# Four groups ahead and four buffers in the attention ahead of two feed-forward stages, with the guard of the row sums on GpSimd

## The reference

```python
k_sum = k.reshape(B, H, nb, block, D).max(axis=3)
v_sum = v.reshape(B, H, nb, block, D).mean(axis=3)
scores_l = where(|i - j| < 16, scale * q @ k.T, -1e9)
scores_s = scale * q @ k_sum.T + log(32)
a = exp(all - max(all)); a = a / (sum(a) + 1e-9)
x = a @ concat(v, v_sum)                 # 1536 tokens x 512
x = relu(x @ w_in) ** 2 @ w_out          # 512 -> 2048 -> 512
h = x @ w2_in
out = (P(h) / (Q(h) + 1e-6)) @ w2_out    # P cubic in h; Q = 1 + |b0||h| + |b1|h*h
```

## Time and profile before

| | before |
|---|---|
| median of 3 runs | 616.96 us (616.08 to 617.96) |
| profiled execution, its own time | 617.14 us |
| its span | 615.4 us |
| PE busy | 582.0 us (95%), 3360 matmuls |
| DVE busy | 444.0 us (72%) |
| ACT busy | 261.3 us (42%) |
| GpSimd busy | 145.1 us (24%) |
| bytes moved | 32.68 MB, of them 0.34 and 0.08 of instructions |

### The profile page before, as it was taken

The page is one execution under the profiler, slowest core; times in us unless marked ns, Lnnn a source line. Parts: engine busy times, 40 slices in busy tenths (PEclk is TensorE's granted clock), DMA queues, the critical chain, the costliest instruction groups (busy, mean ns, idle before and its releaser), DMA issues.

```text
span 615.4 us, 9725 instructions
## 1 busy us (share of the span) xinstructions
PE 582.0 (95%) x3360; PEld 472.8 (77%) x3360; DVE 444.0 (72%) x834; ACT 261.3 (42%) x553; POOL 145.1 (24%) x150
## 2 busy tenths in 40 slices
PE   4788699999999999999999989999999999999995
PEld 3556578888888888888888867788888888888884
DVE  4678787665343233456675699999999999999996
ACT  3778611111031111311111855556766566766564
POOL 5556610000030000210000656522221222221220
PEclk9999999999999999999999999999999999999999
DMA  8788433000000000022333200000100000100001
GB/s 232 212 261 251 129 128 148 0 1 0 1 0 0 0 0 0 0 81 91 103 102 103 69 1 0 1 0 1 68 0 0 0 0 0 68 1 0 1 2 68
DMA packets 12351, 32.68 MB, mean 53 GB/s; under 512 B 1568, under 2 KB 3872, under 8 KB 12320
## 3 DMA queue, kind: packets, MB, share of 16 engines
q1 hardware_dynamic: 12320, 32.25, 16.8%
HBM read 27.92 MB, written 3.15 MB: 50 GB/s over the span
## 4 chain that ended last, share of the span: by engine, by line
PE 47%; DVE 36%; issue 9%; ACT 3%; DMA 2%; DVEq 1%; POOL 1%; SPq 1%; POOLq 0%
PE bank L499 22%; PE bank L544 21%; DVE ratio L927 9%; DVE numer L909 6%; DVE ratio L921 5%; DVE numer L907 5%; DVE ratio L916 5%; DVE hhi L934 4%; ACT prob L617 2%; DMA vwin<-vsum 2%; PE bank L468 1%; PE bank L449 1%; PE bank L485 1%; PE bank L459 1%; SPq L250 1%
## 5 line engine op out<-in xcount | busy, mean ns | idle before, releaser
L499 PE MATMUL bank<-xhi,whi 128*128 (+1 forms) x384 | 150.3, 391 | 0.3 <-DVE wlo L820 0.3
L499 PE MATMUL bank<-xlo,whi 128*128 (+1 forms) x384 | 149.9, 390 | 0.0
L499 PE MATMUL bank<-xhi,wlo 128*128 (+1 forms) x384 | 149.8, 390 | 0.0
L630 ACT ACTIVATE hsq<-bank 128x512 f32<-128x512 f32 x48 | 28.8, 600 | 218.5 <-PE bank L499 218.5
L409 POOL TENSOR_TENSOR denom<-denom,habs 128x512 f32<-128x512 f32 (+1 forms) x49 | 62.3, 1272 | 250.9 <-ACT denom L686 250.9
L499 PEld LDWEIGHTS bank<-xhi,whi 128*128 128x128 f32 x384 | 72.5, 189 | 15.9 <-DVE wlo L820 0.7
L499 PEld LDWEIGHTS bank<-xhi,wlo 128*128 128x128 f32 x384 | 72.3, 188 | 15.1
L499 PEld LDWEIGHTS bank<-xlo,whi 128*128 128x128 f32 x384 | 72.4, 189 | 14.9
L559 PE MATMUL bank<-whi,hhi 128*128 128x512 f32 x192 | 75.9, 395 | 7.6 <-DVE hlo L938 7.6
L559 PE MATMUL bank<-whi,hlo 128*128 128x512 f32 x192 | 74.8, 390 | 0.0
L559 PE MATMUL bank<-wlo,hhi 128*128 128x512 f32 x192 | 74.8, 389 | 0.0
(11 more groups left out here) (65 smaller groups left out, 858.9 us busy)
## 6 DMA issues: line engine op xcount, KB each, us to landing
wraw<-w SPq DMA_DIRECT2D x32, 512.0 KB, 4.1
vwin<-vw SPq DMA_DIRECT2D x8, 576.0 KB, 5.4
kraw<-kT SPq DMA_DIRECT2D x8, 400.0 KB, 6.0
q<-qT SPq DMA_DIRECT2D x8, 384.0 KB, 6.4
out<-osb SPq DMA_DIRECT2D x12, 256.0 KB, 2.1
vwin<-vsum SPq DMA_DIRECT2D x32, 36.0 KB
ca<-coef_a SPq DMA_DIRECT2D x1, 2.0 KB, 10.7
braw<-coef_b SPq DMA_DIRECT2D x1, 1.0 KB, 11.8
```

What stands on the lines that cost most here:

```text
L499: last = mm(hps[j % 2][:, :], W[a][:, j, kt * P:(kt + 1) * P], X[b][:, kt, bass.ds(CH * c, CH)], start=k == 0, stop=k == 3 * KT - 1)
```

## The change

The probability buffers are four, and PE's scores, DVE's masks and ACT's exponentials run four, four and three groups ahead rather than three, three and two. The guard goes from DVE to GpSimd and stands one group further ahead (`guard(G + 3)`), as do `invert(G + 2)`, still on DVE, and `normalise(G + 2)`. There are four buffers of value windows, and the order of SP's transfers is another one. Summaries are computed in the groups that `SUMMARY_AT` lists (1, 3, 5, 8, 11, 14, 17). Key rows are loaded without their zero edges, which DVE writes once, and key 0 comes in three parts. The means are built on ACT. The coefficients are loaded later. The first three weights are split by GpSimd in quarters (w_in part, from group 17 on) and by DVE (w_out part, in the last three groups), and the first two hidden tiles are computed in lots of six matmuls in each of the last four groups. Left out below: the parts of names and waits that only follow from the new counts.

```diff
-DVE_FIRST = 2
...
-P_RING = 3
+P_RING = 4
...
+V_RING = 4
...
+THIRD = S // GPB
+SPLIT_FROM = GROUPS - 7
+SUMMARY_AT = [0, 1, 3] + [GPB * n - 4 for n in range(3, NB)]
...
+    prob = [places[1](f"prob{i}", [P, GU, COLS]) for i in range(P_RING)]
...
-    prob = [area(f"prob{i}", [P, GU, COLS]) for i in range(P_RING)]
...
+    vwin.append(area("vwin3", [COLS, NW, P]))
...
-            sp.dma_start(kraw[n % RING][:, :], kT[n]).then_inc(k_in[n % RING], 16)
+            sp.dma_start(kraw[n % RING][:, BAND:BAND + S], kT[n]).then_inc(k_in[n % RING], 16)
+        def load_k_first(i):
+            sp.dma_start(kraw[0][:, BAND + THIRD * i:BAND + THIRD * (i + 1)],
+                         kT[0][:, THIRD * i:THIRD * (i + 1)]).then_inc(k_first[i], 16)
...
-        load_k(0)
+        load_k_first(0)
+        load_k_first(2)
         load_q(0)
+        load_vwin(0)
         load_k(1)
-        load_vwin(0)
         load_q(1)
+        load_k(2)
         load_vwin(1)
-        load_k(2)
         load_q(2)
-        sp.dma_start(ca[:, :], coef_a.partition_broadcast(P)).then_inc(coef_in, 16)
-        sp.dma_start(braw[:, :], coef_b.partition_broadcast(P)).then_inc(coef_in, 16)
-        spread_summary(0)
         for n in range(NB):
-            if n + 2 < NB:
-                load_vwin(n + 2)
+            if n == 0:
+                load_vwin(2)
+            elif n + RING < NB:
+                load_vwin(n + RING)
             if n + RING < NB:
                 load_k(n + RING)
+            if n == 0:
+                spread_summary(0)
+                load_vwin(RING)
+                spread_summary(1)
+            if n + RING < NB:
                 load_q(n + RING)
             if 2 <= n < 2 + EARLY:
                 load_first(n - 2)
+            if n == 5:
+                sp.dma_start(ca[:, :], coef_a.partition_broadcast(P)).then_inc(coef_in, 16)
+                sp.dma_start(braw[:, :], coef_b.partition_broadcast(P)).then_inc(coef_in, 16)
             if n >= 5:
                 for j in range(EARLY + 2 * (n - 5), min(EARLY + 2 * (n - 4), FT // 2)):
                     load_weights(w1, j, *landing(j))
-            if n + 1 < NB:
-                spread_summary(n + 1)
+            if n == 1:
+                spread_summary(2)
+            if 0 < n and n + 2 < NB:
+                spread_summary(n + 2)
...
+        def guard(G):
+            r = G % P_RING
+            pool.wait_ge(exp_done, G + 1)
+            g.tensor_scalar(guarded[r][:, :], rowsum[r][:, :], 1e-9, None, ALU.add).then_inc(guard_done, 1)
...
+        guard(0)
...
+        guard(1)
...
+        normalise(1, 1)
+        guard(2)
+        def split_in(x):
+            j, part = x // 2, SLOT // 4 * (x % 2)
+            index = slice(None), j, slice(part, part + SLOT // 4)
+            split(index, w_hi_pool, x, w_in_ready)
         for G in range(GROUPS):
...
-            if G + 1 < GROUPS:
-                normalise(G + 1, (G + 1) % P_RING)
-            if n + 2 < NB:
+            if G + 2 < GROUPS:
+                normalise(G + 2, (G + 2) % P_RING)
+            if G == 1:
+                load_windows(2)
+                spread_all(2)
+            if 1 <= n < NB - 2:
                 if gi == 0:
...
                 elif gi == 1:
...
-            x = G - GROUPS + 4
-            if x >= 0:
-                if x == 0:
-                    pool.wait_ge(w_first, 16 * EARLY)
-                if x < 2 * (EARLY - DVE_FIRST):
-                    split(half_slot(DVE_FIRST + x // 2, x % 2), w_hi_pool, x, w_early)
+            if G + 3 < GROUPS:
+                guard(G + 3)
+            x = G - SPLIT_FROM
+            if x == 0:
+                pool.wait_ge(w_first, 16 * EARLY)
+            if 0 <= x < 2 * EARLY:
+                split_in(x)
...
+        def hidden_first(j, kt):
+            pe.wait_ge(w_in_ready, 2 * j + kt // 2 + 1)
+            if kt == 0:
+                pe.wait_ge(s_free, done(2, GROUPS - 1))
+            pe.wait_ge(xlo_done, done(2, XPAIRS - NCH if kt == KT - 1 else NCH * kt))
+            hidden(0, j, j, (kt,))
+        early = {GROUPS - 4: [(0, 0), (0, 1)], GROUPS - 3: [(0, 2), (1, 0)],
+                 GROUPS - 2: [(0, 3), (1, 1)], GROUPS - 1: [(1, 2), (1, 3)]}
...
+        scores(2)
...
-        scores(2)
         for G in range(GROUPS):
...
-            if G + P_RING < GROUPS:
-                scores(G + P_RING)
-            if G % GPB == 0 and G // GPB + 1 < NB:
-                summary(G // GPB + 1)
-            j = G - GROUPS + 2
-            if j >= 0:
-                weights_ready(j)
-                if j == 0:
-                    pe.wait_ge(xlo_done, done(2, XPAIRS - NCH))
-                    pe.wait_ge(s_free, done(2, GROUPS - 1))
-                hidden(0, j, j)
+            for ahead in (3, 4) if G == 0 else (4,):
+                if G + ahead < GROUPS:
+                    scores(G + ahead)
+            for n in range(1, NB):
+                if SUMMARY_AT[n] == G:
+                    summary(n)
+            for j, kt in early.get(G, ()):
+                hidden_first(j, kt)
...
+        act.dma_start(kraw[0][:, BAND + THIRD:BAND + 2 * THIRD], kT[0][:, THIRD:2 * THIRD]).then_inc(k_first[1], 16)
+        a.preload_act_table_set("natural_log_exp_and_others")
+        act.wait_ge(consts, 3)
+        act.wait_ge(means_clear, 1)
+        for j in range(GPB):
+            last = a.copy(means[:, j, 2 * j:2 * j + 2], mean[:, :])
+        last.then_inc(means_done, 1)
...
+        exps(1, 1)
...
-        exps(1, 1)
+        exps(2, 2)
         for G in range(GROUPS):
...
-            if G + 2 < GROUPS:
-                exps(G + 2, (G + 2) % P_RING)
+            if G + 3 < GROUPS:
+                exps(G + 3, (G + 3) % P_RING)
             if G == GROUPS - 2:
...
-            if G % GPB == 0 and G // GPB + 1 < NB:
-                copy_summary(G // GPB + 1)
+            for n in range(1, NB):
+                if SUMMARY_AT[n] == G:
+                    copy_summary(n)
...
+        def split_out(j):
+            raw, hi, lo = (t[:, j, KT * P:] for t in (wraw, whi, wlo))
+            dve.wait_ge(w_first, 16 * EARLY)
+            d.tensor_scalar(hi, raw, 1.0, None, ALU.mult).then_inc(w_out_hi, 1)
+            dve.wait_ge(w_out_hi, j + 1)
+            d.tensor_tensor(lo, raw, hi.bitcast(F32), ALU.subtract).then_inc(w_out_ready, 1)
...
         for G in range(GROUPS):
-            if G + 1 < GROUPS:
-                guard(G + 1)
+            if G + 2 < GROUPS:
+                invert(G + 2)
             if G >= 2:
                 (x_lo if G % 2 else x_hi)(G // 2 - 1)
-            if G + 1 < GROUPS:
-                invert(G + 1)
-            for n in range(2, NB):
-                for part in range(GPB):
-                    if max(GPB * (n - 2) - 1 + part, 0) == G:
-                        block_max(n, part, 1)
-            if G + P_RING < GROUPS:
-                masked(G + P_RING)
-            j = G - GROUPS + 1 + DVE_FIRST
-            if 0 <= j < DVE_FIRST:
-                if j == 0:
-                    dve.wait_ge(w_first, 16 * EARLY)
-                split(j, j)
+            if G == 1:
+                block_max(2, 0, GPB)
+            for n in range(3, NB):
+                part = G - GPB * (n - 2) + 1
+                if 0 <= part < GPB:
+                    block_max(n, part, 1)
+            for ahead in (3, 4) if G == 0 else (4,):
+                if G + ahead < GROUPS:
+                    masked(G + ahead)
+            if G >= GROUPS - EARLY:
+                split_out(G - GROUPS + EARLY)
...
-    arrays = {"qT": features_first(q), "kT": np.pad(features_first(k), ((0, 0), (0, 0), (BAND, BAND))), "vw": windowed(v),
+    arrays = {"qT": features_first(q), "kT": features_first(k), "vw": windowed(v),
...
```

More of the change, by code:

```diff
@@ L165, in build @@
     q_in = [sem(f"q_in{r}") for r in range(RING)]
+    k_first = [sem(f"k_first{i}") for i in range(GPB)]
     k_in = [sem(f"k_in{r}") for r in range(RING)]
-    vw_in = [sem(f"vw_in{r}") for r in range(RING)]
-    vsum_in = [sem(f"vsum_in{r}") for r in range(RING)]
+    vw_in = [sem(f"vw_in{r}") for r in range(V_RING)]
+    vsum_in = [sem(f"vsum_in{r}") for r in range(V_RING)]
     coef_in = sem("coef_in")
@@ L736, in _ @@
         dve.sem_inc(g_ready, 2)
+        for r in range(RING):
+            d.memset(kraw[r][:, 0:BAND], 0.0)
+            last = d.memset(kraw[r][:, BAND + S:], 0.0)
+        last.then_inc(edges, 1)
+        d.memset(means[:, :, :], 0.0).then_inc(means_clear, 1)
         d.memset(one[:, :], 1.0 + 1e-6).then_inc(coef_step, 1)
@@ L750, in make_mask @@
             d.memset(mask[QW:P, 2, KW - BAND:KW], MASKED).then_inc(mask_step, 1)
-        def make_means():
-            d.memset(means[:, :, :], 0.0).then_inc(mask_step, 1)
-            dve.wait_ge(mask_step, 6)
-            dve.wait_ge(consts, 3)
-            for j in range(GPB):
-                last = d.tensor_copy(means[:, j, 2 * j:2 * j + 2], mean[:, :])
-            last.then_inc(means_done, 1)
         def block_max(n, part, parts):
```

(6 more changed lines are left out.)

88 lines of the change are left out of this document (43 added, 45 removed).

## The result

| | before | after |
|---|---|---|
| median | 617.23 us (4 runs) | 623.93 us (4 runs, 619.77 to 626.38) |
| ratio, 95% interval | | 1.0094 (1.0052 to 1.0136) |
| profiled execution | 617.14 us | 619.77 us |
| its span | 615.4 us | 618.0 us |
| output 0 / turn 1 / turn 20 / dense loop | 18.46 / 19.07 / 68.25 / 84.30 us | 23.28 / 24.33 / 76.14 / 86.94 us |

The changed kernel is 0.9% slower; the forecast was 614.4 us, and 623.93 lies outside the range. So does the profiled execution (619.77 us), which is the fastest of the four. A second set of four runs, compared with other runs of the kernel before, gave 622.51 us and a ratio of 1.0048 (1.0030 to 1.0066).

What follows compares the result with a forecast made beforehand. Before the dense loop, attention's ring (4.8 us for two groups) plus DMA waits were taken as the bound, the feed-forward as fixed. 22.1 + 49.2 + 10.3 = 81.6 us, 2.7 earlier than 84.30, gave 614.4 us; range 609.8 to 618.0.

Steps and rivals of the forecast that it cites:

- turn 1: Start of group 1's four transposes on PE (turn G: group G's); forecast at 22.1 us, before at 19.07.
- turn 1 to 5: Early attention groups: output 3 newly waits 2.5 us for the spread of summary 1; 11.1 us in all.
- turn 5 to 17: Middle attention groups: keys issued late behind spreads make two chains of 15.5 us, 31.0 us in all.
- turn 17 to 20: Attention groups without a new key, at the engines' own pace; 6.6 us.
- way out: Turn 20 to the dense loop: earlier weight splits and hidden matmuls in lots of six; 10.3 us, saving 5.75.
- dense loop to the end: Feed-forward stages from the first dense matmul on: length unchanged to 0.3 us.
- First output: Output 0 waits for summary 0's spread, now behind 912 KB more: 2.8 us later, at 21.3 us.
- Clock there: PE starts slowly after waiting for output 0: 0.2 us for turn 1, 0.5 us for the stretch behind it.
- the third rival: PE stays at 1.2 GHz after waiting for the first spread, between turns 1 and 8: 619.0 us; chance 0.14.
- Guard on GpSimd: Guards of 0.17 us leave DVE and take 0.2 us each on GpSimd; nobody on the path waits.
- What the ring gives back, SP's order takes: Attention middle: the four buffers' gain is lost to SP's transfer order; 49.2 us, what it was.
- The ring: Attention's loop of exponentials, guard, normalising, turn and copy: 2.4 us a group before, 1.6 with three in flight.

Runs made afterwards that it cites:

- kernel 1: Changed kernel with the spread of summary 0 issued ahead of value window 2 and key 3; 617.71 us, ratio 0.9966 to the kernel before.
- kernel 3: Changed kernel with 20 unused identity matmuls on PE while it waits ahead of output 0; 623.52 us, ratio 1.0082 to the kernel before.
- kernel 6: Kernel before the change with only the new way out of attention (weight splits, hidden matmuls in lots of six); 615.80 us, ratio 0.9944.
- kernel 9: kernel 4 with each block's weights issued behind its spread instead of between query and key; 613.50 us, ratio 0.9910 to the kernel before.
- kernel 2: Changed kernel with key n+4 issued ahead of the spread of summary n+2; 622.21 us, ratio 1.0048 to the kernel before.
- kernel 4: Changed kernel with the order edits of kernel 1 and kernel 2 together; 616.42 us, ratio 0.9958 to the kernel before.
- kernel 8: Changed kernel with SP's order rewritten (spread 0 first; then key, query, window, spread, weights) and summary 1 in group 0; 617.49 us, ratio 0.9967.
- kernel 10: kernel 9 with summary 1 computed in group 0 and its spread issued ahead of window 3 and key 4; 613.68 us, ratio 0.9928.
- 11: kernel 9 with the guard back on DVE, right ahead of the reciprocal; 614.64 us, ratio 0.9931 to the kernel before.
- kernel 7: kernel 1 with 16 more identity matmuls on PE ahead of output 6 and of output 13; 617.86 us, ratio 0.9989.

## Why the prediction was wrong

Even at a granted clock of 0.999 the kernel took 619.77 us, so the sum of the steps itself came out 5.4 us too low; the lower clock of the other executions came on top. By its own steps, on the axis of the profiled execution:

| step | forecast | measured |
|---|---|---|
| output 0 | 21.3 | 23.28 |
| turn 1 | 22.1 | 24.33 |
| turn 1 to 5 | 11.1 | 11.4 |
| turn 5 to 17 | 31.0 (+ 0.5 clock) | 32.8 |
| turn 17 to 20 | 6.6 | 7.6 |
| way out | 10.3 | 10.8 |
| dense loop to the end | as before | as before |
| time of the profiled execution | 614.4 | 619.77 |

- **"First output" was mis-sized, and it was the largest single error: + 4.8 us, forecast + 2.8.** The mechanism held (kernel 1 takes it away). The 912 KB were priced at the 268 GB/s of the start, but behind 12.5 us DMA moved 209 GB/s at a busy share of 0.92, which makes 4.4 us; and the 0.7 I took off, because before the last issue and output 0 were 2.5 us apart, was a discount without a row for it. That is 2.0 of the 5.4 us. The size isn't sharp: with this start output 0 lay between 21.01 and 24.89 in five profiled executions.
- **"Turn 5 to turn 17" held in kind.** DVE's reduces wait for keys, up to 2.4 us. The first of the two chains came out as written: key 5 issued at 42.30 (turn 5 + 6.6, forecast 6.5), DVE's reduce of it at 47.24, 4.9 later (forecast 5.0), turn 11 at 51.26, 4.0 behind that, in all 15.5 us. The second took 17.2: key 7 was issued at 58.55 (turn 11 + 7.3), took 5.9 us and not 5.0 to land, and turn 17 came 4.0 behind it. So 0.8 are a late issue and 0.9 the landing; for one chain of the two the bound of 6.0 that I had written down would have been right.

```profile
47.24 0.42 DVE L827 TENSOR_REDUCE ksum<-kraw 128x8 f32<-128x256 f32 x1 [1.91 <-DMA kraw<-kT]
```

- **"Turn 17 to turn 20" was 1.0 us short.** I had no new key there, but key 7 reaches in: scores 21, the first of its block, stood 1.08 us for the block's third reduce and GpSimd's copy. The sum had no term for that; scores four groups ahead want the maxima of the next block a group earlier.
- **"Clock there" is the step that failed in kind.** I charged 0.2 and 0.5 us around the first output and looked for the lower clock only between turns 1 and 8 (the third rival, 0.14). The slow start came, larger than that: output 0 to turn 1 took 1.05 us and not 0.61, and turn 1 to turn 2 took 3.61, where the same matmuls at the full clock make about 2.6 (an estimate from their later pitches). It was the harmless place all the same: output 3 waits for its spread behind it anyway, and kernel 3 shows that curing it gains nothing. The clock falls again later, behind waits. In the second profile that happened twice, and turn 1 to turn 20 took 4.4 us more than in the first, where it didn't happen; longer waits for keys (6.8 us, not 5.7) are a part of the 4.4. It fits the median (623.93), 4.2 us above the profiled execution, since the slower three had granted clocks of 0.988 to 0.994; how much of it is the clock alone stays open. The waits of 2 us or more were in the forecast; I didn't ask what PE's clock does behind them, though the earlier trace rows showed a stretch at 0.62 behind a wait.
- **"The way out" held:** 10.8 against 10.3, granted clock 1.00, lots of six; kernel 6 shows most of it alone.
- **"Guard on GpSimd" held:** 0.22 us a piece (taken: 0.2), and no cost of its place in two comparisons.
- **"What the ring gives back, SP's order takes" held in part.** The ring is gone as a bound: where nothing is waited for, groups follow each other at 2.1 us (turns 7 to 11 of kernel 9, 36.67 to 45.11), against 2.4 before. SP's order took that back and more, since three edits of it alone (kernel 9) bring turn 1 to 20 to 49.5 us. But no kernel with four buffers has a shorter middle than those with three (49.2 before, 48.6 in kernel 6), so that the ring's gain can be had at all isn't shown. In kernel 9's profile the dense loop starts at 79.74 us, and in kernel 6's, with three buffers and the new way out alone, at 79.77; of the 5.6 us that kernel 9's ratio makes, kernel 6 has 3.5. That its 613.50 us lie near my 614.4 is chance: the middle is as long as forecast, but not for the reason given.

Left open in part: in kernel 9 turn 1 to 20 (49.5 us) is still no shorter than before (49.2), although the ring of three is gone and DVE waits for no key. PE's stops without a wait (2.8 us in two times) and the spread of output 3 (1.2 us) make 4 us. The slow start adds some 1.6, an estimate (turn 1 to turn 2 took 4.2 us, against 2.6 at the full clock's pitches). And its chain of waits goes through the landing of a query and, in four groups, through ACT's exponentials:

```profile
26.46 5.55 DMA q<-qT
...
49.81 1.51 ACT prob L675 x7
```

The mere bytes aren't the bound of the whole middle: from 28 to 68 us DMA's busy share is 0.72 here, and 0.82 in kernel 6, whose middle is shorter. No run sets the four buffers into SP's old order, so what the ring alone is worth was not measured.

## What to carry to other kernels

When a transfer is put further ahead, list what small transfers now stand behind it, and price the queue at the rate measured in that stretch, not at the best rate of the trace. Price a long wait of PE twice, once as the wait and, as an upper bound, once more as the matmuls behind it at half the clock; single executions will differ in whether the second is paid. A long wait for another engine in a view of waits says only who came last: the guard was waited for 9 to 12 us, and moving it made no difference that the runs could show. Before you look for a gain in one part, run the other part of the change alone: kernel 6 got most of what kernel 9 gets.

## What the runs showed of the hardware

- **PE stopped inside runs of matmuls that have no wait between them**, at the same few places in different kernels: ahead of the last two matmuls of output 13 in kernels 2, 4 and 8 to 11 (0.5 to 1.3 us), behind the fifth or sixth of output 16 in kernels 4 and 8 to 11 (0.5 to 1.7 us), ahead of the last three of scores 23 in kernels 2 and 4 (3.2 and 2.3 us). The two traces of the changed kernel and kernels 1, 6 and 7 have no such stop. In kernel 9:

```profile
53.97 0.33 PE L529 MATMUL bank<-probT,vwin 120*64 120x64 f32 x2 [1.34 <-issue]
...
60.10 0.39 PE L529 MATMUL bank<-probT,vwin 120*64 120x64 f32 x5
...
61.96 0.57 PE L529 MATMUL bank<-probT,vwin 120*64 120x64 f32 x11 [1.47 <-issue]
```

  That it hangs on the place in the program, at times from 60 to 66 us, makes the supply of instructions a suspect; the cause stays open, and no run here tested it. The Trainium skill, "Runtime: NRT & Kernel Launch", section "Instruction fetch mechanics", has each engine's sequencer fetch its instructions in blocks over a DMA queue of its own and calls the crossing of a block mostly hidden. If these stops are such crossings, they were not hidden here.
- **Small transfers didn't pass large ones of the same queue.** 144 KB of spread landed 2.5 us behind its last issue with 3504 KB issued ahead of it since the start, 7.2 us behind it with 4416 KB, and 10 us behind it where 2304 KB had been issued in the 4 us before (kernel 8). The landing is taken as the start of the output that reads it.
- **The granted clock fell to about half inside the attention in nine of the fourteen profiled executions**, behind stretches in which PE had stood: for keys in the changed kernel's second profile (0.85 and 1.71 us of work in 3 us), for spreads in kernels 4 and 8, for a query in kernel 10, behind a stop without a wait in kernel 2. It doesn't always follow: in kernel 4 PE worked 1.04 of the 3 us from 69 to 72, and the clock still read 1.00 there and in the next 3 us. Useless matmuls put into such stretches kept it at 1.00 (kernel 7). It makes a part of what looks like scatter between runs: in kernel 9 the runs at 0.992 to 0.994 took 2.5 us more than those at 0.999.
